# Routing one step behind its rows in an attention and two-layer expert kernel: three entry buffers, an earlier gate, and the gate columns in a run's last step

## What is computed

```python
x = attention(r, k, v, w, u)                      # (3072, 384)
logits = x @ w_gate + modality_bias[modality_id]  # layer 1: one expert
e_idx = argmax(logits); gate_w = softmax(logits)[e_idx]
y[e_idx == e] = gate_w * (relu(x @ w1[e]) @ w2[e])
logits = y @ w_gate2 + log1p(exp(y @ w_noise)) * noise   # layer 2: two experts
top2, top2_w = the two largest of logits, softmax over them
out[rows of e] += top2_w * (relu(y @ w1b[e]) @ w2b[e])
```

## Time and profile before

| | |
|---|---|
| median of 3 runs | 1048.9 us (1048.46 to 1050.92) |
| the profiled execution | 1047.57 us, of it span 1045.9 us |
| busy share of the span | PE 89%, PE weight load 85%, DVE 54%, POOL 40%, ACT 24% |
| mean granted clock | 0.942 |
| chain that ended last | PE 71%, DVE 12%, issue 7%, POOL 4%, DMA 3% |

### The profile page before, as it was taken

How to read it: one execution, slowest core, us unless ns; L and a number is a source line. 1 busy time by engine, 2 the same in 40 slices (tenths; PEclk the granted TensorE clock), 3 DMA queues, 4 the chain that set the end, 5 groups by cost and what they waited for, 6 DMA issues and landing times.

```text
span 1045.9 us, 22934 instructions
## 1 busy us (share of the span) xinstructions
PE 927.8 (89%) x7093; PEld 894.1 (85%) x7094; DVE 564.5 (54%) x1295; ACT 245.9 (24%) x441; POOL 422.4 (40%) x457
## 2 busy tenths in 40 slices
PE   6999998896659989977467899999999999999995
PEld 5888887896659988976367899999999999999995
DVE  8889998481435554576448244443534444443532
ACT  2232242012202322233322022221312222220210
POOL 7333335021335434554434343434433434343333
PEclk9999999896779999998688999999999999999998
DMA  8787898016201111122122343432443534332323
GB/s 266 241 259 254 284 363 298 1 44 202 92 17 33 47 31 31 47 93 87 54 94 84 61 120 93 113 97 51 99 120 77 133 105 105 100 50 38 54 45 47
DMA packets 61785, 115.97 MB, mean 111 GB/s; under 512 B 14320, under 2 KB 42128, under 8 KB 61712
## 3 DMA queue, kind: packets, MB, share of 16 engines
q1 hardware_dynamic: 39552, 75.37, 21.8%
q0 software_dynamic: 18272, 34.89, 15.9%
q10 hardware_dynamic: 3888, 4.80, 1.3%
HBM read 83.62 MB, written 31.51 MB: 110 GB/s over the span
## 4 chain that ended last, share of the span: by engine, by line
PE 71%; DVE 12%; issue 7%; POOL 4%; DMA 3%; DVEq 1%; ACT 1%; SPq 0%; another core or an unknown queue 0%; ACTq 0%; POOLq 0%
PE ps L1850 19%; PE ps L1852 19%; PE ps L1851 19%; PE ps L1797 2%; PE ps L1756 2%; PE ps L1810 1%; PE ps L1752 1%; PE ps L1698 1%; DVE grow L1021 1%; PE ps L1721 1%; POOL lists L619 1%; PE ps L1783 1%; DVE hid_lo L1529 1%; DVE rest L1006 1%; DVE scores L1036 1%
## 5 line engine op out<-in xcount | busy, mean ns | idle before, releaser
L1850 PE MATMUL ps<-x_hi,weights 128*128 128x256 f32 x984 | 284.8, 289 | 20.5 <-DVE x_lo L1524 14.6
L1852 PE MATMUL ps<-x_hi,weights 128*128 128x256 f32 x984 | 283.4, 288 | 2.9 <-issue 2.4
L1851 PE MATMUL ps<-x_lo,weights 128*128 128x256 f32 x984 | 283.5, 288 | 2.6 <-issue 2.5
L1850 PE MATMUL ps<-weights,hid_hi 128*128 (+1 forms) x616 | 221.3, 359 | 16.9 <-DVE hid_lo L1529 15.8
L1851 PE MATMUL ps<-weights,hid_hi 128*128 (+1 forms) x616 | 214.6, 348 | 0.0
L1850 PEld LDWEIGHTS ps<-x_hi,weights 128*128 128x128 f32 x984 | 192.5, 196 | 24.8 <-issue 14.1
L1852 PE MATMUL ps<-weights,hid_lo 128*128 (+1 forms) x616 | 213.1, 346 | 0.0
L1852 PEld LDWEIGHTS ps<-x_hi,weights 128*128 128x128 f32 x984 | 192.7, 196 | 5.5 <-issue 5.5
L1851 PEld LDWEIGHTS ps<-x_lo,weights 128*128 128x128 f32 x984 | 192.6, 196 | 2.4 <-issue 2.2
L920 ACT ACTIVATE hid_hi<-ps 128x512 fp32r<-128x512 f32 x164 | 97.0, 596 | 411.6 <-PE ps L1852 394.3
L1529 DVE SCALAR_TENSOR_TENSOR hid_lo<-ps,hid_hi 128x512 fp32r<-128x512 f32 x164 | 111.8, 689 | 146.2 <-ACT hid_hi L920 115.5
(11 more groups left out here) (309 smaller groups left out, 1162.1 us busy)
## 6 DMA issues: line engine op xcount, KB each, us to landing
stage<-in_w_dram SPq DMA_DIRECT2D x18, 1536.0 KB
kv_in<-in_kv_T_dram SPq DMA_DIRECT2D x24, 512.0 KB, 5.8
kv_in<-in_kv_T_dram SPq DMA_DIRECT2D x24, 448.0 KB, 4.2
w_in<-in_w_T_dram SPq DMA_DIRECT2D x24, 258.5 KB, 4.6
moe_rows<-zeros SPq DMA_DIRECT2D x26, 192.0 KB, 4.1
out_dram<-zeros SPq DMA_DIRECT2D x26, 192.0 KB
x_rows<-y_tok ACTq DMA_DIRECT2D x24, 192.0 KB
w2T_raw<-in_w_T_dram SPq DMA_DIRECT2D x2, 1536.0 KB, 8.1
```

Of the source, the lines that this page charges most:

```text
L1850: pe.matmul(out_ps, hi, by_hi, start=first, stop=False)
L1851: pe.matmul(out_ps, hi, by_lo, start=False, stop=False)
L1852: return pe.matmul(out_ps, lo, by_hi, start=False, stop=final)
```

## The change

Group n is now handled in step n, not in step n+1 (group 1 and the first half of group 2 in step 2). `entry`, `row_at` and `s_listed` exist three times: two by parity, the third for groups 11 and later. The gate factor is computed in step 0 and written before the first step ends; noise 0 and 1 are fetched before the steps. Noise s+1 is fetched in step s up to step 10. In step 11 `early_slots` stands behind `list_rows(11)` and ahead of `scatter(11)`. In a run's last step (`v_now[s] = starts[s+1]`), and no longer in its first, PE makes the next run's columns; SP loads w2 and w1 before w2T. Layer 2's first DVE operation is `row_logits` of the last group, ahead of `split_x(0, ...)`, and that group's `row_ranks` stands between the second and third quarter of up. The spare places of unused list entries become three sets.

```diff
-    NL = NQ + 2 * TS
-    LAG, ONE = 2, 11
-    CUT, EARLY = 9, 2
+    NL = NQ + 3 * 2 * TS
+    ONE = 11
+    CUT, EARLY = 10, 2
...
SP
             with sp.Fori(1, E) as n:
                 with sp.If(n < runs):
+                    load_run(n, lookup(sp, run_expert, n, E - 1))
                     sp.wait_ge(s_vmm, n)
                     sp.nop(nofuse=True)
                     load_w2T(lookup(sp, run_expert, n, E - 1))
-                    load_run(n, lookup(sp, run_expert, n, E - 1))
...
POOL
             def early_slots():
-                pool.wait_ge(s_listed, CUT * 2 * TS * 16)
-                for t in range(TS):
-                    pool.wait_ge(s_scatter[0][0][t], 6 * 16)
-                    pool.wait_ge(s_scatter[0][1][t], 5 * 16)
+                for i in range(2):
+                    pool.wait_ge(s_listed[i], CUT // 2 * 64)
+                    for t in range(TS):
+                        pool.wait_ge(s_scatter[0][i][t], CUT // 2 * 16)
...
-                    if peeled and s == ONE:
-                        early_slots()
...
+                    if peeled and s == 3:
+                        list_rows(2, 1)
+                        gather_noise(3, 1, src_row)
                     rows_read(s + 2)
                     gather(s + 3, 1 - u)
                     if peeled and s == 2:
-                        pool.wait_ge(s_noise, 32)
-                        gather_noise(0, 0, early_src)
-                        gather_noise(1, 1, early_src)
-                    elif peeled and s == 3:
-                        list_rows(1)
+                        list_rows(1, 0)
                         gather_noise(2, 0, early_src)
-                        list_rows(2)
-                        gather_noise(3, 1, src_row)
                     elif late:
-                        list_rows(s)
+                        list_rows(s, 2)
                         gather_noise(s, 2, src_row)
-                    elif not peeled or s > 3:
-                        list_rows(s - LAG + 1)
-                        gather_noise(s, 2 if peeled and s == ONE else u, src_row)
+                    elif peeled and s == ONE:
+                        list_rows(ONE, 2)
+                        early_slots()
+                    elif not peeled or s >= 3:
+                        list_rows(s, 1 - u)
+                        gather_noise(s + 1, 2 if peeled and s == ONE - 1 else 1 - u, src_row)
                     scatter(s, j, u)
-                    if peeled and s == ONE:
-                        list_rows(ONE)
...
                     first_w2()
+                    pool.wait_ge(s_noise, 32)
+                    gather_noise(0, 0, early_src)
+                    gather_noise(1, 1, early_src)
...
ACT
                     if l == 0 and peeled and s == 0:
-                        split_v(0, v0_ps)
-                    if l == 0 and peeled and s == 2:
                         for i in range(2):
                             act.wait_ge(s_xst[i], 16 + 16 * (G // 2))
                         act.wait_ge(s_ask, 1)
                         act.activation(tmp_f[:, :, :], tmp_e[:, :, :], ACT.Exp).then_inc(s_answer, 1)
+                        split_v(0, v0_ps)
...
+                    if l == 0 and peeled and s == 2:
+                        soft_noise(2)
+                        second_weight(2)
                     with act.If(fresh > 0):
...
DVE
-                link(dve.scalar_tensor_tensor(more[:, 0:n], slot_run_f[:, 0:n], last_run[:, 0:1], starts[:, 0:n],
-                                              ALU.is_lt, ALU.mult))
-                link(dve.tensor_copy(v_now[:, :], more[:, 0:n]))
+                dve.tensor_copy(v_now[:, 0:n - 1], starts[:, 1:n])
+                link(dve.memset(v_now[:, n - 1:n], 0))
...
+                if l == 1:
+                    last = rows_done
+                    landed = dve.value_load(after_i[0:1, 0:1], min_val=32, max_val=32 * NS[0])
+                    row_logits(last, 2, 2, landed, dst_row[:, bass.ds(last * TS - TS, TS)], last * TS)
                 split_x(0, 0, 0)
                 split_x(0, 0, 1)
                 if l == 0:
                     first_counts()
+                    dve.tensor_tensor(tmp_e[:, :, :], logits[:, :, :], per_expert(best[:, 0, :]), ALU.subtract)\
+                       .then_inc(s_ask, 1)
                     low_w2(0)
+                    first_gates()
                     low_v(0, v0_ps)
...
                         for q in range(4):
                             if q:
                                 hidden_low(s, q)
+                            if q == 1:
+                                row_second(row[0])
+                            if q == 2 and peeled and s == 2:
+                                row_places(1, 0, 0, row[5], None)
+                                row_logits(2, 1, 1, 32, early_dst[:, TS:2 * TS], 2 * TS)
                             if q == 3:
                                 split_x(s + 1, 1 - u, 0)
...
-                    if peeled and s == ONE:
-                        row_logits(ONE, 0, 6 * 32, dst_row[:, (ONE - 1) * TS:ONE * TS], ONE * TS)
-                        row_first(ONE, 0)
-                        row_second(ONE)
...
PE
                     up(s, 0, run)
+                    up(s, 1, run)
                     if l == 0 and peeled and s == 3:
-                        row_ranks(1)
-                    up(s, 1, run)
+                        row_ranks(2)
+                    if l == 1 and peeled and s == 0:
+                        row_ranks(rows_done)
...
                     up(s, 2, run)
+                    if l == 0 and peeled and s == 2:
+                        row_ranks(1)
                     up(s, 3, run)
...
-                    if l == 0 and late:
+                    down_second(s, 0, run, two)
+                    if l == 0 and (not peeled or s > 2):
                         row_ranks(s)
-                    elif l == 0 and (not peeled or s > 2):
-                        row_ranks(s - LAG + 1)
-                    elif l == 1 and peeled and s == 0:
-                        row_ranks(rows_done)
-                    down_second(s, 0, run, two)
                     down(s, 0, run, 0)
```

More of the change, by code:

```diff
@@ L1590, in first_layer_step @@
                                 low_w1(run + 1, q)
-                        if row:
-                            row_places(row[0], row[1], row[4], row[5], peeled and s == ONE)
+                        if peeled and s == 2:
+                            row_first(2, 1)
+                            row_second(2)
+                        else:
+                            row_places(row[0], row[1], row[2], row[5], row[6], peeled and s == ONE)
                         with dve.If(lookup(dve, v_now, s, 1) > 0):
@@ L1645, in second_layer_step @@
                         row_second(last)
-                        for q in (1, 2, 3):
-                            hidden_low(0, q)
+                        hidden_low(0, 1)
+                        row_places(last, 2, 2, src_row[:, bass.ds(last * TS - TS, TS)], written)
+                        hidden_low(0, 2)
+                        hidden_low(0, 3)
                         split_x(1, 1, 0)
-                        row_places(last, 2, src_row[:, bass.ds(last * TS - TS, TS)], written)
                         split_x(1, 1, 1)
@@ L1943, in slot_step @@
                     down(s, 1, run, 0)
-                    if l == 0 and peeled and s == ONE:
-                        row_ranks(ONE)
                     if l == 1 and peeled and s == 1:
```

111 lines of the change are left out of this document (48 added, 63 removed).

## The result

The changed kernel takes 1017.43 us (median of 1011.21, 1012.12, 1022.74 and 1024.12) where the kernel before takes 1048.68 on the same chip: a ratio of 0.970, 95% interval 0.9619 to 0.9781. The forecast was 1009 in a range of 996 to 1022: the side and the range held, and 40 were forecast where 31 came. The profiled execution is the slowest of the four, 1024.12 with a span of 1022.0.

A forecast was written before the change was run, and what follows sets the result against it. TensorE works most of the span, so time is won where it stands or runs at its lower clock. Terms 59.2 + 18.1 + 107.5 + 23.0 + 61.0 = 268.8 against 308.5; total minus 40 gives 1009 on the median, range 996 to 1022.

The forecast's parts named there:

- step 2: Layer 1: 27.2 us instead of 38.85; no w2T wait or columns, but a new TensorE wait of 7 for row_any.
- step 3: Layer 1: 32.0 us instead of 43.67; late noise 2 causes a wait of 11.5 in place of 21.1.
- step 4: Layer 1: starts without a stop, so 18.1 us instead of 20.08.
- steps 5 to 9: Layer 1 loop: same operations, 1.5 us taken off 8.4 of stops, giving 107.5.
- step 10: Layer 1, last step of the input's first run: columns at the high clock (5.43) fill stops; 23.0 us in the sum.
- 11, 12, change of layer: End of layer 1: POOL's way to noise 12 sets layer 2's start, 61.0 us after step 11's start against 75.5.
- The gate's cover: Gate work in step 0 lies where POOL idles, cost zero; without that cover step 2's gain shrinks by up to 10.
- the forecast case: Whole kernel: about 40 us saved, 1009 on the median, within 1003 to 1015; chance 0.64.
- rival B: POOL chains dearer, early_slots and late entry cost 6 to 10 more, columns at low clock: 1016 to 1026; chance 0.17.
- A: Rival: POOL chains cheaper, noise 2 back in time or early_slots free: about 997, or 985 with both; chance 0.15.
- D: Rival: POOL becomes the bound of every step, since list_rows(s) waits for its own step's row_places: 1055; chance 0.03.
- C: Rival: step 10 keeps 6.2 of stops and gets 5.4 of columns on top: plus 4, 1013; inside the forecast's spread.

The follow-up runs named there:

- the load's version: Changed kernel with SyncE's w1 load for layer 2's second expert waiting until the early rows land; chip C: 1034.94 against 1066.02, ratio 0.971.

## Why the prediction was right, and where its sum was off

The stretches, forecast and measured, in us (before to after where there is a pair):

| stretch | forecast | A | D | B, after |
|---|---|---|---|---|
| step 2 | 27.2 | 38.9 to 27.9 | 38.2 to 27.6 | 27.1 |
| step 3 | 32.0 | 43.7 to 33.3 | 43.4 to 34.7 | 34.7 |
| step 4 | 18.1 | 20.1 to 24.1 | 22.4 to 24.1 | 18.2 |
| steps 5 to 9 | 107.5 | 109.1 to 108.1 | 117.5 to 119.3 | 91.0 |
| step 10 | 23.0 | 21.4 to 26.7 | 24.4 to 27.7 | 20.8 |
| 11, 12, change of layer | 61.0 | 75.5 to 60.3 | 75.6 to 61.1 | 58.1 |
| sum | 268.8 | 308.5 to 280.3 | 321.5 to 294.5 | 249.9 |

- **Step 2** was right: 27.9 for 27.2, the wait for row_any 6.95 for 7, no wait for w2T. The gate's cover was priced at up to 10; taken away it cost 12.2 on the medians, 14.7 in step 2.
- **Step 3** was right in its mechanism and 1.3 too short on A, 2.7 on B and D. The term was noise 2's way: forecast 41.3 from step 2's start to the landing, measured 42.7 (278.47 - 235.78); from there to down 7.7 for 6.6. The main thing in it: DVE's low_w2 and POOL's operations had been priced as if each ran alone, and POOL's copy behind the split took 1.72 for 0.19, until low_w2 was done. (The prediction's own terms, 253.8 + 3.45 + 11.7, also give 269.0 and not its 269.4.) The stop is 13.3 for 11.5.
- **Step 4** was the step that failed: 24.1 for 18.1. The prediction took the earlier trace rows's third window, 20.08 busy throughout at a clock of 0.89, turned it into 17.9 at full clock, and took that for the price of a step without a stop. On B that price is real (18.16). But in A's step 4 TensorE is busy 20.87 at a clock of 0.93 and stands 3.2, of them 1.64 for hid_lo and the rest in pauses of issue. On A, C and D its issue pauses in nearly all loop steps, in both kernels, and steps 4 and 5 of the kernel before on A (20.08 and 20.09) were the exception, not the rule. Why isn't known: that the stop of 8.6 ahead of step 4 gave the issue time to run ahead was my guess, but the kernel before on C has the same stop and 24.5 for the step.
- **Steps 5 to 9** were right: 108.1 for 107.5.
- **Step 10** was 3.7 too short. The term was mainly the clock of the columns: their 8.4 (440.86 to 449.24), 3.0 over the 5.43 taken, lies between the two prices of the earlier trace rows, and the dearer one was kept for the range only. On D the columns took 7.2, so that they explain only 1.7 of the 4.7 by which that step is over the forecast; on B 5.7.
- **Steps 11, 12 and the change of layer** were right in what sets their end, 60.3 for 61.0: POOL's way to noise 12 ended at 55.3 after step 11's start for 56 (early_slots took 11.9 for 11.2). Step 11 itself was not "a plain step, 18.3": it took 23.1 on A, 23.6 on D, 19.5 on B. The products of step 12 ended 2.8 later than walked, which only made the stop behind them shorter, 16.7 for some 20. That the total came out right there is luck as far as TensorE's part goes.
- **What lies ahead of step 2**, +6.1, was no term at all: it goes with the granted clock of that execution (0.88 against 1.00 from 150 to 185, 0.82 against 0.88 in steps 0 and 1), and the gate's work there costs nothing on D.
- Layer 2 is 1.8 shorter (505.9 for 507.7), forecast 0.5.

These deviations add up: 0.7 + 1.3 + 6.0 + 0.6 + 3.7 - 0.7 + 6.1 - 1.3 = 16.4, of which 6.1 and part of step 10 go with this execution's clock: the median is 6.7 below the profiled run, and 8.4 above the forecast.

The median lies 2.4 above the forecast case's own 1015 and inside rival B's 1016 to 1026: of what B named, the dearer chains of steps 2 and 3 came with 2 to 3, the columns more than halfway to the low clock; most of the rest is step 4, which no rival named. That the time still lies in the range is in part the range's width, and not a cause that was foreseen. A didn't come. D didn't come: in steps 5 to 9 POOL is busy 52.2 of 108.1. C's price came, but not for its reason: the columns do fill the stops of step 10. By undoing parts on their own: the early gate 12.2, the columns 0, the two further entry buffers 0. What is left, the order of rows and lists, was not undone by itself, and it is the larger part: 30 of the 42.3 on B. For it there are the traces of both kernels on A and D, in which the stops at row_any, x_lo and ahead of layer 2 are smaller or gone in the same places; that is an argument from before and after, not an experiment on this part alone.

The Trainium skill (ScalarE: Activation LUTs, "What ACT_TABLE_LOAD costs") gives each switch of tables a drain of about 1.38 us on top of its load; for the four switches in step 2 that would be 5 to 6, an estimate. The trace speaks against it: step 2 came out 0.7 from a sum without any drain, the load at 255.90 begins 0.02 after the function ahead of it ends, and the function behind the load of 254.37 begins at 255.66, 0.01 after that load's 1.28.

Open: why step 4 of the changed kernel is dearer than before on A, and why the change wins 42.3 on chip B and 31 to 32 on A, C (the load's version) and D. There is no trace of the kernel before on B, so how its loop steps ran there isn't known.

## What to carry to other kernels

When a buffer's wait is gone, ask which order of the queue made it: here one buffer did as well as three once the writes were issued in their own step, as its wait of 5.7 lay under a longer one; and the next gain was two calls moved ahead of a split on one queue. Price a step from several of its kind, and put the granted clock beside each duration: a single step that looks clean may be the exception. A part that fills another wait is worth nothing until that wait is shortened, so the parts of a change are to be undone one at a time.

## What the runs showed of the hardware

- **VectorE and GpSimd take turns.** With POOL's split from 256.00 to 259.51, low_w2 ran from 255.97 to 261.12: it ended 1.61 after the split, about its own length of 1.76. On chip A 261.64 to 265.43 beside a split that ended at 263.82 leaves 1.61 again. A copy of 128x8, 0.17 alone, ended at 263.20 beside a split that ended at 263.17. It goes the other way too: POOL's copy of 0.19 took 1.72 on chip A (263.77 to 265.49) and 1.70 on chip B (259.46 to 261.16), until low_w2 was done (265.43 and 261.12). By the rule of the Trainium skill (SBUF — State Buffer, "SBUF: two separate sides") a VectorE operation with two inputs in SBUF and a GpSimd operation that reads SBUF exclude each other for a whole instruction; the trace agrees for low_w2 and the split. The prediction had priced POOL's issue beside DVE (2.26 for 0.95), and not these waits.
- **The price of a loop step goes with the chip** (or with the occasion, which the runs can't tell from it). Steps 5 to 9 of the changed kernel take 18.2 us each on B, 21.6 on A, 23.8 on C (the load's version) and 23.9 on D, and within 0.4 of that in the kernel before where both were traced (A, C, D). Of the 17.0 that the five steps take more on A than on B, 9.0 are pauses of issue between matmuls (0.2 to 0.9 each) and 8.0 lie in busy time at a clock of 0.97 for 1.00; of the 28.2 on D 12.1 are standing and 16.1 busy time at 0.91. The cause of the pauses wasn't tried.
- **Mean granted clock and time go together on some chips:** about 10 us for 0.01 on A and B, some 3 us for 0.009 on D. Runs of one kernel on one chip differ by 0.003 to 0.015. Medians over several runs are needed for a few us; one profile isn't enough.
- **A large load just ahead of a small gather.** On chip B the gathered rows landed after 6.9 and 7.4 in the two traces in which the 1.5 MB load was issued 1.1 ahead of the last gather, and after 2.1 in the two in which it came after; on A, C and D it always came after, and they landed after 2.1 to 2.5. No edit isolated it.
